# An attention and two-layer network kernel on one core: both key halves of an item's scores in one visit of TensorE

## The reference, cut to what matters

```python
scores = scale * np.matmul(q, k.transpose(0, 1, 3, 2))      # q, k, v: (4, 8, 576, 64), float32
kth = np.partition(scores, -32, axis=-1)[..., -32:-31]
scores = np.where(scores >= kth, scores, -1e9)              # the 32 largest of each row stay
attn = softmax(scores)                                      # minus the row's maximum, exp, over sum + 1e-9
x = np.matmul(attn, v)                                      # to (2304, 512)
h = x @ w_in;  g = np.maximum(0.01 * h, h);  x = g @ w_out  # 512 -> 2048 -> 512
h = x @ w_in2; g = 0 | (h + 1)**2 / 4 | h for h <= -1, between, >= 1; out = g @ w_out2
```

## Time and profile before

| | |
|---|---|
| median of 3 runs | 1298.22 us (1291.61 to 1299.02) |
| profiled execution: its time, its span | 1297.69 us, 1295.9 us |
| TensorE busy | 1167.3 us (90%), 8128 matmuls |
| VectorE, ScalarE, GpSimd busy | 71%, 55%, 50% |
| granted TensorE clock, mean | 0.958 of full |
| chain that ended last | TensorE 63%, ScalarE 9%, GpSimd 7%, VectorE 5%, DMA 5% |

### The profile page before, as it was taken

The page is one execution under the profiler, slowest core; times in us unless marked ns, Lnnn a source line. Parts: engine busy times, 40 slices in busy tenths (PEclk is TensorE's granted clock), DMA queues, the critical chain, the costliest instruction groups (busy, mean ns, idle before and its releaser), DMA issues.

```text
span 1295.9 us, 22677 instructions
## 1 busy us (share of the span) xinstructions
PE 1167.3 (90%) x8128; PEld 1016.4 (78%) x8128; DVE 917.2 (71%) x2080; ACT 708.7 (55%) x1665; POOL 647.9 (50%) x662
## 2 busy tenths in 40 slices
PE   3434799889999989999999999999998999999998
PEld 1222687768888878888888778888878999999898
DVE  7979577988889999899988997988998110001111
ACT  4646575656567656566666765656567442233430
POOL 5557654864357443465434653634368262134641
PEclk9966798889999999999999999999998999999999
DMA  9678788777666768767766655333332446445352
GB/s 338 230 283 286 247 299 274 238 235 264 196 204 204 240 202 282 267 220 239 247 229 224 203 186 184 115 115 114 104 111 96 143 146 205 162 163 169 125 180 101
DMA packets 80032, 261.52 MB, mean 202 GB/s; under 512 B 8881, under 2 KB 12977, under 8 KB 79921
## 3 DMA queue, kind: packets, MB, share of 16 engines
q1 hardware_dynamic: 71856, 244.35, 56.0%
q10 hardware_dynamic: 8064, 15.73, 3.4%
HBM read 221.77 MB, written 38.27 MB: 201 GB/s over the span
## 4 chain that ended last, share of the span: by engine, by line
PE 63%; ACT 9%; POOL 7%; DVE 5%; DMA 5%; issue 3%; SPq 0%; ACTq 0%
PE ps_f L678 48%; PE ps_av L643 6%; PE ps_s L601 4%; POOL gate L529 4%; DMA w_split<-w_ring 4%; PE ps_t L620 2%; DVE top L874 2%; ACT part_o L796 2%; ACT gate L807 2%; PE ps_t L626 1%; ACT part_r L795 1%; ACT probs L747 1%; DVE part_r L901 1%; POOL part_o L535 1%; DVE work L877 1%
## 5 line engine op out<-in xcount | busy, mean ns | idle before, releaser
L678 PEld LDWEIGHTS ps_f<-gate,w_ring 128*128 128x128 f32 x3072 | 417.9, 191 | 48.0 <-issue 25.3
L678 PE MATMUL ps_f<-gate,w_ring 128*128 128x288 f32 (+2 forms) x3072 | 438.8, 301 | 17.4 <-POOL gate L529 16.5
L874 DVE MAX8 top<-work 128x8 f32<-128x576 f32 x432 | 309.6, 744 | 0.0
L514 POOL TENSOR_TENSOR drop<-scores,drop 128x576 f32<-128x576 f32 x144 | 206.9, 1437 | 96.8 <-DVE drop L883 96.8
L678 PE MATMUL ps_f<-xy_even,w_ring 128*128 128x288 f32 (+2 forms) x1536 | 228.5, 304 | 5.9 <-DMA w_ring<-w_split 5.0
L678 PEld LDWEIGHTS ps_f<-xy_even,w_ring 128*128 128x128 f32 x1536 | 211.4, 193 | 27.8 <-issue 20.1
L678 PE MATMUL ps_f<-xy_odd,w_ring 128*128 128x288 f32 (+2 forms) x1536 | 220.2, 299 | 3.8 <-ACT part_o L796 1.8
L678 PEld LDWEIGHTS ps_f<-xy_odd,w_ring 128*128 128x128 f32 x1536 | 206.4, 189 | 19.5 <-issue 10.8
L877 DVE MATCH_REPLACE8 work<-top,work 128x576 f32<-128x576 f32 x288 | 213.4, 741 | 0.0
L529 POOL TENSOR_TENSOR gate<-part_r,gate 128x288 fp32r<-128x288 f32 (+2 forms) x128 | 103.9, 814 | 183.4 <-ACT gate L800 183.0
L901 DVE SCALAR_TENSOR_TENSOR part_r<-part_r 128x288 f32<-128x288 f32 (+2 forms) x128 | 70.5, 551 | 131.9 <-ACT part_o L796 131.4
(11 more groups left out here) (63 smaller groups left out, 1342.0 us busy)
## 6 DMA issues: line engine op xcount, KB each, us to landing
w_ring<-w_split SPq DMA_DIRECT2D x363, 512.0 KB, 4.2
w_split<-split SPq DMA_DIRECT2D x43, 512.0 KB, 3.3
raw<-wd SPq DMA_DIRECT2D x43, 256.0 KB, 3.8
w_split<-w_ring SPq DMA_DIRECT2D x21, 512.0 KB, 6.2
kq<-kqd ACTq DMA_DIRECT2D x12, 576.0 KB, 5.5
direct_raw<-wd SPq DMA_DIRECT2D x21, 256.0 KB, 6.4
v_sb<-vd ACTq DMA_DIRECT2D x12, 320.0 KB, 4.4
kq<-kqd SPq DMA_DIRECT2D x4, 576.0 KB, 7.2
```

The source lines that it names most:

```text
L514: pool.tensor_tensor(slot, scores[:, it.n % S_SLOTS, t - it.first, :], slot, ALU.add).then_inc(masked, 1)
L678: mm = pe.matmul(bank(u), ww, xx, start=a == 0, stop=a == count - 1)
L874: dve.max(top[:, t % T_SLOTS, 8 * r:8 * r + 8], source(t, r)).then_inc(dve_step, 1)
```

## The change

- **Scores.** `score(it)` makes both key halves in one visit, in step `first`. Half 0 goes to `ps_s`, half 1 to the two banks of `ps_t`. If transposes are due in the same step (`scores_first`), the visit stands at the step's start; if not, behind `first`. ScalarE's two copies (`copy_scores`) move the same way.
- **Waits.** The visit waits until all transposes of earlier steps have been copied (`p_t_copied`, `ITEMS_OUT`), and a transpose until all scores made so far have been copied (`scores_copied`, `ITEMS_SCORED`).
- **Pair results of the first chunk.** `copy_values` and `low_x` of groups 0 to 3 move into the next step: behind `exponential` (before the weights' split) and behind `mask`; for group 3 to the start of step 22.
- **Sums.** `close_sum` and `invert_sum` of group 3's two items come one tile earlier in VectorE's program.

```diff
+def item_closing(t):
+    for it in ITEMS:
+        if it.last + INV_LAG - (it.gp == CHUNKS[0].last_gp) == t:
+            return it
+ITEMS_OUT = [sum(o.last + OUT_LAG < it.first for o in ITEMS) for it in ITEMS]
+ITEMS_SCORED = [sum(o.first <= it.last + OUT_LAG for o in ITEMS) for it in ITEMS]
...
+        ps_half = [ps_s, ps_t[:, :, :].rearrange("p (a c) n -> p a (c n)", a=2)]
...
-                need(pe, scores_copied, 2 * it.n + j)
+                need(pe, scores_copied, 2 * it.n)
+                need(pe, p_t_copied, ITEMS_OUT[it.n])
...
+                for j, out in enumerate(ps_half):
...
             def transpose(it):
                 pe.wait_ge(probs_ready, it.n + 1)
+                pe.wait_ge(scores_copied, 2 * ITEMS_SCORED[it.n])
...
-                if it:
-                    score(it, s - it.first)
+                it = item_starting(s)
+                if it and scores_first(s):
+                    score(it)
                 for u in first:
                     feed(u)
-                if it and it.mixed:
-                    score(it, 1)
+                if it and not scores_first(s):
+                    score(it)
...
+                for gp in values_at(s - 1, True):
+                    if s == READY[0]:
+                        copy_values(gp)
+                if it and (quiet or scores_first(s)):
+                    copy_scores(it)
...
                 if closed:
                     exponential(s - EXP_LAG)
+                for gp in values_at(s - 1, True):
+                    if s != READY[0]:
+                        copy_values(gp)
...
-                if not quiet and it and it.mixed:
-                    copy_scores(it, 1)
+                if it and not quiet and not scores_first(s):
+                    copy_scores(it)
...
-                shut = ITEM_OF[t - INV_LAG] if 0 <= t - INV_LAG < TILES else None
-                if shut and shut.last != t - INV_LAG:
-                    shut = None
+                shut = item_closing(t)
```

More of the change, by code:

```diff
@@ L308, in values_at, with item_starting, item_done, scores_first @@
             if (t + OUT_LAG == s if quiet else t + AV_LAG == s) and quiet != any(PLAN[t + OUT_LAG])]
+def item_starting(s):
+    it = ITEM_OF[s] if s < TILES else None
+    return it if it and it.first == s else None
+def item_done(s):
+    it = ITEM_OF[s - OUT_LAG] if 0 <= s - OUT_LAG < TILES else None
+    return it if it and it.last == s - OUT_LAG else None
+def item_closing(t):
+    for it in ITEMS:
+        if it.last + INV_LAG - (it.gp == CHUNKS[0].last_gp) == t:
+            return it
+    return None
+def scores_first(s):
+    return item_done(s) is not None
+ITEMS_OUT = [sum(o.last + OUT_LAG < it.first for o in ITEMS) for it in ITEMS]
+ITEMS_SCORED = [sum(o.first <= it.last + OUT_LAG for o in ITEMS) for it in ITEMS]
 def need(eng, sem, value):
@@ L575, in _ @@
                         low_direct(a)
+                for gp in values_at(s - 1, True):
+                    if s == READY[0]:
+                        low_x(gp)
                 for u in first:
@@ L585, in _ @@
                     event(u)
-                for gp in values_at(s, False) + values_at(s, True):
+                for gp in values_at(s, False):
                     low_x(gp)
@@ L592, in _, with score @@
         def _(pe):
-            def score(it, j):
-                if j == 0 and it.rows in (0, 2):
+            def score(it):
+                if it.rows in (0, 2):
                     pe.wait_ge(kq_loaded[it.pair], 16 * (it.b + 1))
-                need(pe, scores_copied, 2 * it.n + j)
+                need(pe, scores_copied, 2 * it.n)
+                need(pe, p_t_copied, ITEMS_OUT[it.n])
                 q, k = kq[:, it.pair, 0:S], kq[:, it.pair, S:2 * S]
[L598 to L602, removed]
-                              start=True, stop=True).then_inc(scores_done, 1)
[L604 to L612, removed]
@@ new lines, in score @@
+                for j, out in enumerate(ps_half):
+                    c0, c1 = j * PART, (j + 1) * PART
+                    if not it.mixed:
+                        rows = slice(it.rows * P, (it.rows + 1) * P)
+                        pe.matmul(out[:, 0, 0:PART], q[0:D, rows], k[0:D, c0:c1], start=True, stop=True)
+                        pe.matmul(out[:, 1, 0:PART], q[D:P, rows], k[D:P, c0:c1],
+                                  start=True, stop=True).then_inc(scores_done, 1)
+                        continue
+                    rows = slice(MAIN, S)
+                    if j == 0:
+                        pe.matmul(out[D:P, 1, 0:PART], q[D:P, rows], k[D:P, REST:REST + PART], start=True, stop=True)
+                    else:
+                        pe.matmul(out[D:P, 1, 0:PART - REST], q[D:P, rows], k[D:P, REST + PART:S], start=True, stop=True)
+                        pe.matmul(out[D:P, 1, PART - REST:PART], q[D:P, rows], k[D:P, 0:REST], start=True, stop=True)
+                    pe.matmul(out[0:D, 0, 0:PART], q[0:D, rows], k[0:D, c0:c1],
+                              start=True, stop=True).then_inc(scores_done, 1)
@@ L694, in _ @@
                     feed(u)
-                done = ITEM_OF[s - OUT_LAG] if 0 <= s - OUT_LAG < TILES else None
-                if done and done.last == s - OUT_LAG:
-                    transpose(done)
+                if item_done(s):
+                    transpose(item_done(s))
                 for u in third:
@@ L830, in _ @@
             for s, (first, second, third) in enumerate(PLAN):
[L831 to L832 removed]
+                it, done = item_starting(s), item_done(s)
                 closed = ITEM_OF[s - EXP_LAG] if 0 <= s - EXP_LAG < TILES else None
@@ L837, in _ @@
                         high_direct(a)
-                if it:
-                    copy_scores(it, s - it.first)
-                if quiet and it and it.mixed:
-                    copy_scores(it, 1)
-                if done and done.last == s - OUT_LAG:
+                for gp in values_at(s - 1, True):
+                    if s == READY[0]:
+                        copy_values(gp)
+                if it and (quiet or scores_first(s)):
+                    copy_scores(it)
+                if done:
                     normalise(done)
-                if quiet and done and done.last == s - OUT_LAG:
+                if quiet and done:
                     copy_transposed(done)
@@ L851, in _ @@
                     event(u)
-                if not quiet and it and it.mixed:
-                    copy_scores(it, 1)
+                if it and not quiet and not scores_first(s):
+                    copy_scores(it)
                 for u in second:
                     event(u)
-                for gp in values_at(s, False) + values_at(s, True):
+                for gp in values_at(s, False):
                     copy_values(gp)
-                if not quiet and done and done.last == s - OUT_LAG:
+                if not quiet and done:
                     copy_transposed(done)
```

20 lines of the change are left out of this document (10 added, 10 removed).

## The result

The changed kernel takes 1306.47 us (median, 1303.81 to 1307.16) where the kernel before took 1296.02 us beside it: ratio 1.0077, interval 1.0055 to 1.0098, some 10 us slower. The profiled span went from 1295.9 to 1304.8 us. The work of TensorE did shrink: busy 1147.7 us instead of 1167.3. Its waits grew by more.

A forecast was written before the change was run, and what follows sets the result against it. TensorE's work plus its idle time bounds the kernel, its savings counting in 7 of 10 places; -7.6 + 7.3 + 2.7 - 5.5 + 1.5 + 1.3 = -0.3 us gives 1297.4 us, range 1285 to 1308.

The forecast's parts named there:

- Fewer visits: TensorE from step 21 on: 68 second score visits go, 10.9 us, at the chain's 70% 7.6 us saved.
- leaving costs nothing to be seen: TensorE's score visits: only entering costs, 0.17 us from a unit; the second pass takes 0.34 us as the first.
- fourth rival: TensorE's visits: leaving costs as much as entering, hidden in the last pass; 8 us more saved, 1289 us; chance 0.10.
- The waits that go: TensorE at and after mixed items: waits for score copies, 15.8 us in all, of which 5.5 us are won.
- fifth rival: Mixed items: the waits move whole to the transposes, nothing won of 15.8 us; 1303 us; chance 0.08.
- ScalarE's term: ScalarE in steps with transposes and a visit: both score copies now precede normalising; costs 1.5 us.
- The new wait: TensorE's visits behind transposes wait for their copy: 7.3 us at seven of 11 places, 2.7 us at 202 us.
- second rival: ScalarE late at the copies: each of 11 places costs 3 us, 33 instead of 10 us; 1320 us; chance 0.08.
- The quiet phase: Stretch up to 137.68 us, idle for TensorE, its length counting in full: first unit 1.3 us later.
- The sums: VectorE near 106 us: sums a tile earlier wait some 6 us, absorbed by tile 20's slack; costed at nothing.
- third rival: VectorE bound at the start: the early sums' 6 us aren't absorbed; 1303 us; chance 0.09.
- the first (1272 us): Everything hidden: three waits vanish whole and units cover the copies' wait; 1272 us; chance 0.07.

The follow-up runs named there:

- six late visits: Changed kernel with the score visit behind the first unit at six places where transposes stand in the step before: 1298.33 us, ratio 1.0032 to the kernel before.
- best kernel: Changed kernel with halves scored separately, sums and pair results as before in the quiet phase, and nine visits behind the first unit: 1286.02 us, ratio 0.9938.
- tail experiments: Kernel before with extra score visits between units after the attention, results unused: 60 single ones 1339.14 us, 30 double ones 1330.88 us, one execution each.
- nine late visits: Changed kernel with the score visit behind the first unit at all nine places directly behind transposes of the step before: 1292.47 us, ratio 0.9978.
- scores-alone kernel: Changed kernel with only the score part, pair results and sums of the first chunk back in their old places: 1307.61 us, ratio 1.0085.
- the moves alone: Kernel before with pair results and sums moved as in the change, scores as before: 1298.48 us, ratio 1.0013.

## Why the prediction was wrong

The forecast was -0.3 us, the result about +10. The wide range (to 1308 us) held it and within 1% was right, but it lies outside the 1291 to 1304 us that had the chance of 0.58, and the way was wrong: the forecast was none to slightly faster. The ratios split it, the first line with some 2.7 us of uncertainty, the others, each a difference of two ratios, with some 4:

| part | forecast | measured |
|---|---|---|
| one visit from step 22 on, no place collides, quiet phase as before | -7.6 - 5.5 + 1.5 = -11.6 | -8.0 (last but one experiment; by spans -12.2) |
| quiet phase with sums and pair results | +1.3 | +5.2 (0.9938 to 0.9978; by spans 6.9; with six late visits 8.5, by spans 3.9) |
| visits directly behind transposes | +7.3 + 2.7 = +10.0 | +12.8 (0.9978 to 1.0077; by spans 14.2) |

By the ratios all three lines missed in the same direction, by 3.6, 3.9 and 2.8 us. That the first came out as near as it did is luck: fewer visits saved 24.5 us of TensorE instead of 7.6, and the waits, taken together, grew by 12.6 us in the best kernel instead of falling by 5.5, both off by some 17 us in opposite directions. The steps that failed are the waits that were to go, the order of two DMA issues in the quiet phase, put at nothing, and the number of places at which the new wait counts.

**Fewer visits: -7.6 was mis-sized.** A merge saves 0.36 us of TensorE, not 0.17, shown by the tail experiments. For 68 merges that is 24.5 us of work, if the 32 that don't lie between units save as much. It can be checked: the span less the first unit's start and TensorE's waits from 146 us on is 1111.9 us before and 1087.4 in the best kernel, 24.5 less. The step "leaving costs nothing to be seen" failed: I read the equal pitch of the first and the second pass as the pitch of the work, but a half has only those two passes, one with a part of the entry in it and one with the exit. The fourth rival's mechanism, a price of leaving hidden in the last pass, stood. Its time, 1289, did not come, since waits grew with it. The Trainium skill, TensorEngine Tiling (Array Packing), Key Properties, says that a change of the tiling mode drains TensorE. The trace agrees in that both borders of a visit cost time, 0.36 us for the pair; that all of it is this drain isn't shown, since transposes, in the units' own mode, cost 0.08 us to enter too.

**The waits that go: -5.5 was nothing.** This is the step that failed by the most. The fifth rival came, and more of it: the waits moved, to gates and normalised tiles ahead of the transposes. In the best kernel TensorE waits 58.9 us from 146 us on (its whole list), in the kernel before 46.3: 12.6 more, although 15.8 us at L609 and L601 are gone. -24.5 + 12.6 = -11.9 us is near the -12.2 of the spans. Those for gates grew from 16.5 to 24.2 us, those for normalised tiles from 3.5 to 11.8: I had let TensorE save 2.5 us at 458 us, but its next unit hangs on ScalarE's gate, which comes behind four copies. Moving all copies took the gates' wait down to 14.0 us and that for tiles to 0.4, so the block of copies did feed them. But in both orders tried the copies must be done before TensorE can go on, since the transposes need the bank: 44.0 and 27.7 us of wait came in their place. ScalarE's term of +1.5 us was the small view of the same thing.

**The new wait: +10.0 became about 13 to 14.** The mechanism was right and the wait at a place nearly so (1.37 us at 430 and 473 us where I had 1.07 to 1.30); the count was too low. All eleven places wait (the two with a unit between by 0.46 and 0.58 us), 15.7 us in sum, and not the seven and the one at 202 us; that one cost 3.35 us where I took 2.7. The six and the nine late visits showed that these places are the loss. They cost more than their wait: from the changed kernel to nine late visits all waits together fell by 9.4 us (67.8 to 58.4), and TensorE's time outside its waits by another 6.4 (1093.0 to 1086.6), less 1.6 for a later first unit. The second rival (1320 us) would have needed 3 us a place.

**The quiet phase: +1.3 was too little, for a reason I had put down as nothing.** "Their issue times shift with the quiet phase" was said of SyncE's queue; in the scores-alone kernel a prefetch and a raw load change places, 0.6 us apart, and 4 of the 5 us come from that (5.00 us of wait instead of 1.00). The load landed after 6.0 to 7.4 us in all seven kernels that issued it behind the prefetch (those that score the quiet phase in one visit), after 3.1 to 4.0 in the six that issued it ahead, and after 3.2 in the changed kernel with the prefetch moved. There the first unit came only 1.35 us earlier, because the moved pair results and sums delay it too: in the kernel before with the moves alone the load landed after 3.4 us, and the first unit still came at 142.47, 4.8 us late, beside 142.68 with the prefetch moved. So by these traces, which agree to 1 or 2 us, either cause delays the first unit by some 5 us, and both together by 6.35. I had put the moved copies at a delay of 0.66 us and the order at nothing. That the delay is absorbed in the DMA-paced stretch holds for the kernel before with the moves alone (0.7 of 4.8 us left) and not for the merged visits: from nine late visits to the best kernel the first unit comes 8.2 us earlier and tile 31 of VectorE 8.9 us. Why one kernel absorbs the delay and the other doesn't is open.

**The sums: nothing, as forecast.** VectorE's wait of 7.68 us was there (forecast some 6) and taken up later. The third rival is out, and so is the first (1272 us), which had all waits vanish.

**What stays open.** Of the changed kernel's 8.9 us of longer span, -24.5 + 21.5 us (waits 46.3 to 67.8) + 6.35 (first unit) make 3.4; some 5.5 us are left. They go with the nine visits behind transposes: TensorE's time outside its waits is 1111.9 us before, 1093.0 in the changed kernel, and 1086.6 once those visits are moved. A lower granted clock is a likely cause (its mean over 500 to 750 us was 1.00 before, 0.98 in the changed kernel and 0.99 with nine late visits; the visit at 473.40 us ran at 0.50), a dearer change from transposes to a visit another; no experiment separates them.

## What to carry to other kernels

When a merge puts data into banks that another product uses, list every place where the two uses meet in consecutive steps and move one of them behind work that has nothing to do with either: that was worth 13 us here. What an engine pays to enter and leave a mode can't be read from a stretch in which every piece touches a border; it takes one with a piece in the middle. And a phase whose length counts in full is worth keeping as it was: two DMA issues that changed places there cost 4 us of waiting.

## What the runs showed of the hardware

A 256 KB load issued 0.6 us behind a 576 KB prefetch from another engine's queue landed after 7.4 us (the scores alone) and made its consumer wait 5.00 us; issued 0.8 us ahead of it, it landed after 4.0 us and the wait was 1.00 us (the kernel before). A 64-row score visit between 128-row units costs 0.36 us of TensorE beyond its passes of 0.24 us: 0.15 ahead of the first pass, 0.11 in the first and 0.10 in the last. After the wait of 4.03 us that ended at 468.94 us the granted clock was 0.50 until 476 us, the lower of the levels of 1.2 and 2.4 GHz: the two groups of transposes started 0.85 us apart where 0.43 is usual, and the passes of the visit at 473.40 us 0.48 us apart instead of 0.24, so that the visit took 2.2 us instead of 1.17.
